# Clustered attention, mixture of experts and MLP: a new order of the work in the expert tiles

## The chip, the core and the metric

The kernel runs on one core of a Trainium2 chip. Its engines are TensorE (PE, matmuls and transposes), VectorE (DVE), ScalarE (ACT), GpSimd (POOL) and SyncE (SP), which here only issues DMAs. Each engine works through its own list of instructions in order, and semaphores tie the lists together. The metric is the time of one execution on the device in microseconds (us), as a median of several runs; lower is better.

## The reference

Three layers follow each other, all in float32.

```python
# 1. attention, B=2 H=8 S=768 D=64, 16 clusters: a query sees only keys of its own cluster
q_assign = argmax(einsum(q_n, c_n)); k_assign = argmax(einsum(k_n, c_n))
scores = where(q_assign[..., None] == k_assign[..., None, :], scale * q @ k.T, -1e9)
x = softmax(scores) @ v                  # -> (1536 tokens, 512)
# 2. mixture of experts, E=8, hidden 1024, one expert per token
e_idx = argmax(x @ w_gate, axis=1); gate_w = softmax(x @ w_gate)[e_idx]
eom = sigmoid(x @ w_output_gate)[e_idx]
for e in range(E):
    out[mask] = gate_w * eom * (maximum(x[mask] @ w1[e], 0) @ w2[e])
# 3. MLP, hidden 2048
h = out @ w_in
return (h * sigmoid(1.702 * h)) @ w_out
```

## The kernel before, in words

**Precision.** Each float32 operand of a large matmul is split into a high part in the fp32r format and a low part (the rest). One product is three matmuls: low times high, high times low, high times high. ScalarE (`*_high`, `high`, and `split_*` for weights) makes the high parts, VectorE (`*_low`, `low`, and its own `split_*`) the low ones.

**Attention** takes the first 296 us. It also computes the gate logits. As soon as the first batch's six columns of 128 tokens are done, they are given to experts; the other six follow in two stages of three columns at the end (`STAGES`). `choose(st, ...)` picks each token's expert on VectorE; `ranks(st)` on TensorE counts, with small bf16 matmuls (L785), how many tokens ahead of this one go to the same expert; `place(st)` on VectorE (L1441) turns that into the row `pos`. GpSimd then writes the rows of `x` to their places in DRAM, `xs` (`place_rows`, indirect DMAs), and token number and gate scale to `row_info` (`place_info`, L601). Every expert has a region of its own in `xs`.

**Tiles.** An expert's rows are worked on in tiles of 128. The numbers of tiles are known only at run time (`ntiles`). Since a region's last tile is not full, SyncE writes 128 rows of zeros behind its last row (`fill(e)`, L468); a fetch of rows by ScalarE for expert e + 1 waits for that expert's zeros (`s_pad`, L1169).

**The loop.** `expert_loop` (L345) writes out for each expert a body for its first tile (k = 0), one for its second (k = 1, under an If), and a loop for the further ones (k = 2, under an If). `only(e)` runs, in place of the second body, where an expert has one tile. TensorE, ScalarE, VectorE and SyncE each run this structure with their own `expert_tile(p, e, k)`. A call works at two tiles: it finishes tile p and starts tile g = p + 1.

On TensorE (L948) a tile is: `down(p, ., 0)` (6 matmuls of the second layer), `tile_transpose(g)` (4 transposes of the fetched rows `xg`), `down(p, ., 2)` (6), `hidden_transpose(p, 1)` (4 transposes of the hidden rows), a wait for `xtl_done`, `hidden(g, e, 0)` (12 matmuls), `down(p, ., 4)` and `(p, ., 6)` (12), `hidden_transpose(g, 0)` (4), `hidden(g, e, 1)` (12) and `turned(p)` (4 transposes of the scaled output).

On ScalarE (L1199) it is: two loads of row numbers, `tile_high(g)`, `fetch` of the rows after (a DMA), `high(p, 1)`, `relu(g, 0)`, two weight splits, `scaled(p)` (output times gate scale), `high(g, 0)`, two splits, `relu(g, 1)`, `turned_high(p)`. VectorE follows with the low parts (L1594). The splits are of the second weights of the same expert in the first tile, and of the first weights of the next expert in the second; `first_of_next` does the latter for an expert with one tile.

**Weights.** SyncE fetches 1 MB pieces into `raw`, which shares its memory with `wl`; in an expert's first tile it waits until the last tile of the expert before is through with its first weights (`h_ready`), then `fetch_first(e + 1)`, and until it is through with the second (`y_ready`), then `fetch_second(e + 1)` (L487). Before the loop SyncE does, in order: `fill(0)`, wait for the dispatch, rows of tile 1, `fill(1)`, wait for `g_rows` (the row numbers `tile_row`), `fetch_second(1)`, `fill(2)`.

**GpSimd** reads one tile's scales per tile from `row_info` (L675), the first after all of `place_info` has landed.

**The MLP** runs from about 532 us to the end in three groups of 512 tokens.

## Time and profile before

| | |
|---|---|
| median of 3 runs | 807.75 us (807.22 to 811.66) |
| the profiled execution | 811.05 us, its span 809.6 us |
| TensorE busy | 750.1 us, 93% of the span |
| VectorE, ScalarE, GpSimd busy | 425.4, 371.3, 164.5 us |
| chain that ended last | PE 70%, ACT 6%, DVE 6%, issue 4%, DMA 4%, SP queue 4%, POOL 3% |
| read from DRAM, written | 56.01 MB, 9.05 MB |

The profile lists every instruction with its engine and its line in the code. Matmuls overlap each other, so a matmul of 0.39 us that starts 0.23 us after the one before costs 0.23: read the distance between starts. Times in the rows are in us from the start of the span. A bracket after a row gives how long the engine had been idle and what it then waited for.

### The profile page before, as it was taken

Reading aid. Unit: us, or ns where it says so; the run is one execution under the profiler, and the core shown is the slowest. Engines: PE = TensorE matmul, PEld = TensorE weight load, DVE = VectorE, ACT = ScalarE, POOL = GpSimd, SP = SyncE. Lnnn points to the kernel's source line nnn. Section 1 sums busy time; section 2 is a strip of 40 time slices with the busy share of each in tenths; the row PEclk is TensorE's granted clock in tenths of the full one; section 3 lists DMA queues with packets and bytes.
Section 4 is the critical chain, followed back from the end, with each engine's and each line's share of the span. In section 5 each row is a group of like instructions: output and inputs, shape, how many; then the busy total and the mean of one; then the engine's idle time right before and its main releaser. Section 6 shows DMA issues by size and latency. Waiting matters only on the chain.

```text
span 809.6 us, 11950 instructions
## 1 busy us (share of the span) xinstructions
PE 750.1 (93%) x4099; PEld 640.2 (79%) x4099; DVE 425.4 (53%) x791; ACT 371.3 (46%) x707; POOL 164.5 (20%) x253
## 2 busy tenths in 40 slices
PE   4799999999999997679999999999999999999994
PEld 3699899988988875468777878878888888888883
DVE  4587888879878866246464646454322212221221
ACT  2577777777776854256565656463201110110110
POOL 5232242222625874101010101010000100020001
PEclk9999999999999999879999999999999999999998
DMA  8672552835526534864655465160000100010001
GB/s 178 149 173 67 133 124 64 185 70 132 138 68 138 211 116 120 248 236 140 238 179 188 136 217 209 39 208 2 1 0 7 46 0 1 1 53 0 1 1 52
DMA packets 61331, 86.36 MB, mean 107 GB/s; under 512 B 32577, under 2 KB 34769, under 8 KB 60753
## 3 DMA queue, kind: packets, MB, share of 16 engines
q1 hardware_dynamic: 55728, 75.23, 32.9%
q0 software_dynamic: 3376, 6.35, 2.2%
q10 hardware_dynamic: 2160, 3.93, 1.8%
q8 instruction: 38, 0.62, 0.3%
q14 instruction: 29, 0.23, 0.1%
HBM read 56.01 MB, written 9.05 MB: 80 GB/s over the span
## 4 chain that ended last, share of the span: by engine, by line
PE 70%; ACT 6%; DVE 6%; issue 4%; DMA 4%; SPq 4%; POOL 3%; ACTq 2%; another core or an unknown queue 0%; DVEq 0%; POOLq 0%
PE ps L982 16%; PE ps L697 8%; PE ps L997 5%; PE ps L998 5%; PE ps L999 5%; PE ps L770 4%; PE ps L912 4%; PE ps L914 3%; PE ps L913 3%; SPq L399 3%; PE ps L899 2%; PE ps L747 2%; PE ps L901 2%; PE ps L900 2%; PE ps L743 2%
## 5 line engine op out<-in xcount | busy, mean ns | idle before, releaser
L1375 DVE TENSOR_TENSOR pt_l<-ps,pt_h 128x384 fp32r<-128x384 f32 x192 | 105.9, 552 | 41.7 <-ACT pt_h L1086 40.5
L1244 ACT ACTIVATE g<-ps 128x512 f32<-128x512 f32 x48 | 28.7, 598 | 205.4 <-PE ps L982 205.4
L1628 DVE CAST gt_h<-g 128x512 fp32r<-128x512 f32 x48 | 20.5, 427 | 179.7 <-ACT g L1244 179.7
L1086 ACT CAST pt_h<-ps 128x384 fp32r<-128x384 f32 x192 | 92.6, 483 | 43.9 <-PE ps L697 43.8
L697 PE MATMUL ps<-ident,probs 128*128 128x128 f32 x576 | 97.3, 278 | 3.5 <-DVE pt_l L1375 1.9
L1334 DVE TENSOR_REDUCE nmax<-ps 128x1 f32<-128x768 f32 x96 | 91.0, 948 | 7.6 <-PE ps L747 7.6
L1057 ACT ACTIVATE probs<-ps,nmax 128x768 f32<-128x768 f32 x96 | 87.6, 913 | 4.8 <-DVE nmax L1334 4.8
L697 PEld LDWEIGHTS ps<-ident,probs 128*128 128x128 f32 x576 | 70.7, 144 | 17.6 <-DVE pt_l L1375 4.3
L982 PE MATMUL ps<-x2t_h,wl 128*128 128x512 f32 x192 | 74.9, 390 | 0.3 <-DVE wl L1545 0.3
L997 PE MATMUL ps<-wh,gt_l 128*128 128x512 f32 x192 | 74.8, 390 | 0.0
L982 PE MATMUL ps<-x2t_h,wh 128*128 128x512 f32 x192 | 74.7, 389 | 0.0
L999 PE MATMUL ps<-wh,gt_h 128*128 128x512 f32 x192 | 74.7, 389 | 0.0
L982 PE MATMUL ps<-x2t_l,wh 128*128 128x512 f32 x192 | 74.7, 389 | 0.0
L998 PE MATMUL ps<-wl,gt_h 128*128 128x512 f32 x192 | 74.7, 389 | 0.0
L770 PE MATMUL ps<-pt_h,vs 128*128 128x384 f32 x192 | 72.7, 379 | 0.0
L899 PE MATMUL ps<-wh,ht_l 128*128 128x512 f32 x128 | 54.9, 429 | 11.2 <-DVE ht_l L1497 6.1
L770 PE MATMUL ps<-pt_l,vs 128*128 128x384 f32 x192 | 64.7, 337 | 0.0
L912 PE MATMUL ps<-wh,xt_l 128*128 128x512 f32 x128 | 53.3, 416 | 7.0 <-DVE xt_l L1491 6.6
L743 PE MATMUL ps<-ka,qa 128*128 128x384 f32 x192 | 58.1, 384 | 1.2 <-DMA kb<-lo_t 1.2
L1545 DVE TENSOR_TENSOR wl<-raw,wh 128x1024 fp32r<-128x1024 f32 x36 | 42.6, 1221 | 25.6 <-ACT wh L1155 25.6
L1540 DVE TENSOR_TENSOR wl<-raw,wh 128x1024 fp32r<-128x1024 f32 x36 | 42.6, 1220 | 24.3 <-ACT wh L1150 24.1
L747 PE MATMUL ps<-kb,qb 80*128 80x384 f32 x192 | 50.8, 346 | 3.0 <-DMA kb<-onehot_t 3.0
(198 smaller groups left out, 1451.6 us busy)
## 6 DMA issues: line engine op xcount, KB each, us to landing
raw<-in_moe_w SPq DMA_DIRECT2D x32, 1024.0 KB, 7.9
ka<-hi_t SPq DMA_DIRECT2D x32, 192.0 KB
raw<-in_moe_w_in SPq DMA_DIRECT2D x4, 1024.0 KB, 5.8
raw<-in_moe_w_out SPq DMA_DIRECT2D x4, 1024.0 KB, 6.7
xg<-xs ACTq DMA_DIRECT2D x15, 256.0 KB
qn<-in_q SPq DMA_DIRECT2D x16, 192.0 KB, 3.6
kn<-in_k SPq DMA_DIRECT2D x16, 192.0 KB, 3.9
vn<-in_v SPq DMA_DIRECT2D x8, 384.0 KB, 5.0
```

What stands on the lines that cost most here:

```text
L697: return nc.tensor.transpose(dst, src, ident[0:src.shape[0], :] if src.shape[0] < P else ident[:, :])
L743: nc.tensor.matmul(ps[:, bank + half, 0:GQ], qa[par][h][:, rows], ka[par][h][:, half * GQ:(half + 1) * GQ], start=True, stop=False)
L770: last = nc.tensor.matmul(ps[:, 6, 0:GQ], vs[par][:, h * T + c, :], src[gp][:, c, :], start=(c == 0 and src is pt_h), stop=(c == T - 1 and ...
L912: nc.tensor.matmul(ps[:, half, :], xt_l[:, c, :], wh[slot][:, w], start=(c == 0), stop=False)
L982: last = nc.tensor.matmul(ps[:, f % 2, :], a[c // 2][:, w], b[:, c, cols], start=first, stop=(c == DC - 1 and a is wh and b is x2t_h))
L997: nc.tensor.matmul(ps[:, 4 + j, :], gt_l[f % 2][:, tok], wh[slot][:, w], start=(f == 0), stop=False)
L998: nc.tensor.matmul(ps[:, 4 + j, :], gt_h[f % 2][:, tok], wl[slot][:, w], start=False, stop=False)
L999: last = nc.tensor.matmul(ps[:, 4 + j, :], gt_h[f % 2][:, tok], wh[slot][:, w], start=False, stop=(f == FC2 - 1))
L1057: nc.scalar.activation(probs[s % 2][:, :].rearrange("p (a n) -> p a n", a=2), halves(score_bank(s)), ACT.Exp, bias=nmax[:, s % 4:s % 4 + 1 ...
L1086: nc.scalar.copy(pt_h[g % 2][:, half * GT:(half + 1) * GT, t3 * P:(t3 + 1) * P], ps[:, 4 + half, 0:GQ].rearrange("p (c n) -> p c n", c=GT) ...
L1334: nc.vector.reduce_max(nmax[:, s % 4:s % 4 + 1], halves(score_bank(s)), AX.XY, negate=True).then_inc(m_ready, 1)
L1375: nc.vector.tensor_tensor(pt_l[g % 2][at_p], ps[:, 4 + half, 0:GQ].rearrange("p (c n) -> p c n", c=GT), pt_h[g % 2][at_p].bitcast(F32), AL ...
```

## The change

- `expert_loop` has an argument `alike`. TensorE sets it: its k = 1 body goes, and one loop handles all tiles after an expert's first. The other engines keep their structure.
- In TensorE's tile `hidden_transpose(p, 1)` moves up behind `tile_transpose(g)`; `hidden_transpose(g, 0)` and `turned(p)` stand together in the middle of `hidden(g, e, 1)`. The two tiles ahead of the loop are reordered likewise. One more `tile_transpose` stands behind the loop.
- ScalarE and VectorE do `tile_high(g + 1)` and `tile_low(g + 1)` as the last operations of a tile, not the first; the weight splits and `turned_*` are placed anew.
- SyncE issues `fill(0)` to `fill(2)` together and every later one an expert earlier; `fetch_second(1)` no longer waits for `g_rows`.
- `ranks` counts only within a stage. What earlier stages add (and region start and gap) is carried in `offset` by VectorE and added in `place` as a second product.

```diff
-        def expert_loop(eng, counter, tile, only=None):
+        def expert_loop(eng, counter, tile, only=None, alike=False):
...
+                if e and not alike:
                     with eng.If(n > 1):
                         tile(eng.snap(counter), e, 1)
                         eng.reg_add(counter, counter, 1)
-                with eng.If(n > 2):
-                    with eng.Fori(2, n):
+                done = 1 if e and alike else 2
+                with eng.If(n > done):
+                    with eng.Fori(done, n):
                         tile(eng.snap(counter), e, 2)
                         eng.reg_add(counter, counter, 1)
...
             sp.wait_ge(g_filled, 1)
-            fill(0)
+            for e in range(3):
+                fill(e)
             sp.wait_ge(s_pad[0], 16)
             sp.wait_ge(s_disp, 16 * NT)
             sp.dma_start(xg[:, :], xs[TILE:2 * TILE, :]).then_inc(xg_in, 16)
-            fill(1)
             sp.wait_ge(pv_done, PAIRS * NG)
-            sp.wait_ge(g_rows, 1)
             fetch_second(1)
-            fill(2)
+            fill(3)
...
                 if k == 0:
-                    if e + 2 < E:
-                        fill(e + 2)
+                    if e + 3 < E:
+                        fill(e + 3)
...
-                nc.tensor.matmul(dst, ones[:, :], region_b[:, 0:n, :].rearrange("p t e -> p (t e)"), start=True, stop=False)
-                if st:
-                    nc.tensor.matmul(dst, ones[0:1, :], gap_b[0:1, :, :].rearrange("p t e -> p (t e)"), start=False, stop=False)
-                for d in range(a + n - 1, 0, -1):
-                    skip = max(0, d - a)
-                    nc.tensor.matmul(dst[:, skip * E:], ones[:, :], picked[:, (a + skip - d) * E:(z - d) * E], start=False, stop=False)
-                nc.tensor.matmul(dst, before[:, :], picked[:, a * E:z * E], start=False, stop=True).then_inc(g_rank, 1)
-                if st != 1:
-                    for t in range(z):
...
+                nc.tensor.matmul(dst, before[:, :], picked[:, a * E:z * E], start=True, stop=False)
+                for d in range(1, n):
+                    last = nc.tensor.matmul(dst[:, d * E:], ones[:, :], picked[:, a * E:(z - d) * E], start=False, stop=(d == n - 1))
+                last.then_inc(g_rank, 1)
+                for t in range(a, z):
+                    last = nc.tensor.matmul(total_of(st), ones[:, :], pick_b[:, t, :], start=(t == a), stop=(t == z - 1))
+                last.then_inc(g_total, 1)
...
             hidden(0, 0, 0, 3)
-            hidden(0, 0, 1, 0, 1)
+            hidden(0, 0, 1, 0, 2)
             hidden_transpose(0, 0)
-            hidden(0, 0, 1, 1)
+            hidden(0, 0, 1, 2)
             down(0, 0, 0)
             hidden_transpose(0, 1)
             down(0, 0, 2)
             down(0, 0, 4)
+            tile_transpose(1)
             down(0, 0, 6)
-            turned(0)
-            tile_transpose(1)
             pe.wait_ge(xtl_done, 2)
             hidden(1, 0, 0)
-            hidden(1, 0, 1, 0, 1)
+            hidden(1, 0, 1, 0, 2)
             hidden_transpose(1, 0)
-            hidden(1, 0, 1, 1)
+            turned(0)
+            hidden(1, 0, 1, 2)
...
                 g, ep = p + 1, e if k else e - 1
                 down(p, ep, 0)
                 tile_transpose(g)
+                hidden_transpose(p, 1)
                 down(p, ep, 2)
-                hidden_transpose(p, 1)
                 pe.wait_ge(xtl_done, g + 1)
                 hidden(g, e, 0)
                 down(p, ep, 4)
                 down(p, ep, 6)
+                hidden(g, e, 1, 0, 2)
                 hidden_transpose(g, 0)
-                hidden(g, e, 1)
                 turned(p)
-
-            expert_loop(pe, tiles, expert_tile)
+                hidden(g, e, 1, 2)
+
+            expert_loop(pe, tiles, expert_tile, alike=True)
...
             down(last, E - 1, 0)
+            tile_transpose(total)
             down(last, E - 1, 2)
...
                 row, ahead_row = row_at(p + 1), region_row_of(g + 1)
-                tile_high(g)
                 fetch(ahead_row, min(e + 1, E - 1))
                 high(p, 1)
-                relu(g, 0)
                 if k < 2:
                     split(whose, 0)
                     split(whose, 1)
+                relu(g, 0)
+                if k < 2:
+                    split(whose, 2)
                 scaled(p)
                 high(g, 0)
+                turned_high(p, row)
                 if k < 2:
-                    split(whose, 2)
                     split(whose, 3)
                 relu(g, 1)
-                turned_high(p, row)
+                tile_high(g + 1)
...
                 row = row_at(p + 1)
-                tile_low(g)
                 low(p, 1)
                 if k < 2:
                     split(whose, 0)
                     split(whose, 1)
+                    split(whose, 2)
                 low(g, 0)
+                turned_low(p, row)
                 if k < 2:
-                    split(whose, 2)
                     split(whose, 3)
-                turned_low(p, row)
+                tile_low(g + 1)
```

Ahead of the loop ScalarE and VectorE are reordered in the same sense: `tile_high(1)` stands before `scaled(0)`, `tile_low(1)` before the gates, and `tile_high(2)`, `tile_low(2)` at the end.

## Rows read from the trace of the kernel before

**Rows 1.** The page, part 1: busy us, share of the span, instructions.

```profile
PE 750.1 (93%) x4099; PEld 640.2 (79%) x4099; DVE 425.4 (53%) x791; ACT 371.3 (46%) x707; POOL 164.5 (20%) x253
```

**Rows 2.** Timeline of TensorE, 320 to 376: start, us, engine, line, operation, output, input, shape, count.

```profile
339.95 0.80 PE L899 MATMUL ps<-wh,ht_l 128*128 128x512 f32 x1 [6.06 <-DVE ht_l L1497]
...
345.24 0.82 PE L697 MATMUL ps<-ident,h 128*128 128x128 f32 x4
...
354.24 0.77 PE L899 MATMUL ps<-wh,ht_l 128*128 128x512 f32 x1 [4.98 <-issue]
...
369.00 0.60 PE L697 MATMUL ps<-ident,y 128*128 128x128 f32 x4
```

**Rows 3.** Timeline of ScalarE, 270 to 385.

```profile
338.59 0.58 ACT L1145 CAST ht_h<-ps 128x512 fp32r<-128x512 f32 x1 [8.47 <-DMA xs<-zeros]
```

**Rows 4.** Timeline of SyncE's DMA issues, 270 to 560.

```profile
310.68 0.35 SPq L477 DMA_DIRECT2D xg<-xs  x1
...
320.65 0.93 SPq L440 DMA_DIRECT2D raw<-in_moe_w  x2
322.48 4.23 SPq L471 DMA_DIRECT2D xs<-zeros  x2
```

**Rows 5.** DMA queues in 350 to 352: queue, packets, MB, share.

```profile
q8 instruction: 1, 0.02, 3.0%
```

**Rows 6.** Timeline of VectorE: start of the experts, expert 1's end, a steady tile.

```profile
311.95 0.69 DVE L1497 TENSOR_TENSOR ht_l<-ps,ht_h 128x512 fp32r<-128x512 f32 x1 [2.15 <-ACT ht_h L1145]
...
314.47 1.22 DVE L1540 TENSOR_TENSOR wl<-raw,wh 128x1024 fp32r<-128x1024 f32 x1
...
350.94 4.63 DVE L1540 TENSOR_TENSOR wl<-raw,wh 128x1024 fp32r<-128x1024 f32 x4
...
413.28 0.69 DVE L1491 TENSOR_TENSOR xt_l<-ps,xt_h 128x512 fp32r<-128x512 f32 x1 [2.05 <-ACT xt_h L1134]
```

**Rows 7.** Windows of 5 us: length, busy time of each engine, granted clock, DMA share, GB/s.

```profile
340.00:345.00 5.00, 5.00 (x12) 3.98 (x13) 2.36 (x2) 1.55 (x2) 0.74 (x2) 0.50 0.60 239
```

**Rows 8.** Timeline of TensorE, steady tiles and the last ones.

```profile
378.73 0.39 PE L901 MATMUL ps<-wh,ht_h 128*128 128x512 f32 x1
378.96 0.60 PE L697 MATMUL ps<-ident,h 128*128 128x128 f32 x4
379.31 0.48 PE L912 MATMUL ps<-wh,xt_l 128*128 128x512 f32 x1
379.63 0.40 PE L913 MATMUL ps<-wl,xt_h 128*128 128x512 f32 x1
...
399.54 0.60 PE L697 MATMUL ps<-ident,h 128*128 128x128 f32 x4
...
410.86 0.60 PE L697 MATMUL ps<-ident,xg 128*128 128x128 f32 x4
...
414.03 0.50 PE L912 MATMUL ps<-wh,xt_l 128*128 128x512 f32 x1 [0.75 <-DVE xt_l L1491]
...
529.02 0.60 PE L697 MATMUL ps<-ident,y 128*128 128x128 f32 x4
...
534.52 0.50 PE L982 MATMUL ps<-x2t_h,wl 128*128 128x512 f32 x1 [0.32 <-DVE wl L1545]
```

**Rows 9.** Timeline of ScalarE, 378 to 427.

```profile
400.18 0.59 ACT L1145 CAST ht_h<-ps 128x512 fp32r<-128x512 f32 x1 [0.71 <-PE ps L697]
...
409.75 0.59 ACT L1160 CAST x2t_h<-ps 128x512 f32 x1
412.66 0.58 ACT L1134 CAST xt_h<-ps 128x512 fp32r<-128x512 f32 x1 [2.32 <-issue]
```

**Rows 10.** Timeline of TensorE, 293.5 to 320.

```profile
319.21 0.50 PE L912 MATMUL ps<-wh,xt_l 128*128 128x512 f32 x1 [1.62 <-DVE xt_l L1491]
```

**Rows 11.** Timeline of GpSimd, 270 to 385.

```profile
339.60 0.59 POOL L675 DMA_DIRECT2D scale<-row_info  x1 [14.54 <-issue]
```

**Rows 12.** DMA issues of the whole span: count, KB each, median us to landing.

```profile
scale<-row_info POOLq DMA_DIRECT2D x16, 1.0 KB, 4.1
```

More of the change, by code:

```diff
@@ L97, in clustered_attention_moe_mlp @@
         first_rows = sb("first_rows", [P, 2, NROWS])
-        region_b = sb("region_b", [P, T, E], BF16)
+        offset = sb("offset", [P, 3, E])
         thresholds = sb("thresholds", [P, NTHR])
@@ L269, in clustered_attention_moe_mlp @@
         g_count = sem("g_count")
+        g_offset = sem("g_offset")
         g_first = sem("g_first")
@@ L1182, in _ @@
             high(0, 1)
-            for i in range(1, 4):
-                split_first(1, i)
+            split_first(1, 1)
+            tile_high(1)
             scaled(0)
+            act.wait_ge(g_region, 1)
+            fetch(region_row_of(2), 1)
+            split_first(1, 2)
+            relu(1, 0)
+            high(1, 0)
             act.wait_ge(s_disp, 16 * NT)
             turned_high(0, 0)
-            tile_high(1)
-            act.wait_ge(g_region, 1)
-            fetch(region_row_of(2), 1)
-            relu(1, 0)
-            high(1, 0)
+            split_first(1, 3)
             relu(1, 1)
+            tile_high(2)
             act.wait_ge(g_tiles, 1)
@@ L1237, in _ @@
             wait_apart(act, xg_in, 16 * total + 16)
-            wait_apart(act, xtl_done, total)
+            wait_apart(act, xtl_done, total + 1)
             for m in range(NMG):
@@ L1436, in total @@
             def total(st):
-                dve.wait_ge(g_total, 1 + st // 2)
-                nc.vector.tensor_copy(count[:, 1:SEG], ps[:, 7, TOTAL:TOTAL + E]).then_inc(g_count, 1)
+                dve.wait_ge(g_total, st + 1)
+                if st < 2:
+                    nc.vector.tensor_tensor(offset[:, st + 1, :], offset[:, st, :], total_of(st), ALU.add).then_inc(g_offset, 1)
+                if st:
+                    nc.vector.tensor_tensor(count[:, 1:SEG], count[:, 1:SEG], total_of(st), ALU.add).then_inc(g_count, 1)
+                else:
+                    nc.vector.tensor_copy(count[:, 1:SEG], total_of(st)).then_inc(g_count, 1)
             def place(st):
@@ L1445, in place @@
                 bank, at_c = (5, (st - 1) * GT * E) if st else (7, 3 * P)
+                if st:
+                    dve.wait_ge(g_offset, st)
+                    dve.wait_ge(g_first, 1)
+                dve.wait_ge(g_pick, st + 1)
+                nc.vector.tensor_tensor(rank[:, own, 1, :], offset[:, st, :].unsqueeze(1).to_broadcast([P, n, E]), pick_b[:, own, :], ALU.mult)
                 dve.wait_ge(g_rank, st + 1)
@@ L1462, in first_gap @@
                 link(nc.vector.tensor_scalar(gap[:, 1:2], gap[:, 0:1], 0.0, None, ALU.max), g_step)
-                nc.vector.tensor_copy(gap_b[:, :, 0:1], gap[:, 1:2].unsqueeze(1).to_broadcast([P, GT, 1])).then_inc(g_first, 1)
+                nc.vector.tensor_tensor(offset[:, 1, 0:1], offset[:, 1, 0:1], gap[:, 1:2], ALU.add).then_inc(g_first, 1)
             def gate(b, part):
@@ L1574, in _ @@
             split_first(1, 0)
+            tile_low(1)
+            split_first(1, 1)
             gate(1, 0)
             gate(1, 1)
-            turned_low(0, 0)
-            tile_low(1)
             dense_rows()
-            split_first(1, 1)
             split_first(1, 2)
             low(1, 0)
+            turned_low(0, 0)
             split_first(1, 3)
+            tile_low(2)
             dve.wait_ge(g_tiles, 1)
```

20 lines of the change are left out of this document (9 added, 11 removed).

## The prediction

> **What bounds the kernel now.** I read the page first. TensorE is busy for 93% of the span [rows 1], so the time is TensorE's own work plus the places where it waits, and only those two can change. The windows and the timeline of TensorE over the experts (296 to 534 us) then show three kinds of lost time.
>
> First, two holes early on: 6.06 us before the matmul at 339.95 and 4.98 us before the one at 354.24 [rows 2]. The first is a chain through a DMA. TensorE wants ht_l from VectorE, which wants ht_h from ScalarE, and ScalarE stood 8.47 us at the fetch of the next rows, held by the zero rows that pad expert 2's region [rows 3]. SyncE issued that pad at 322.48, behind the 2 MB of expert 1's second weights, which went out at 320.65 because they waited for tile_row [rows 4]. The second hole is put down to "issue": VectorE and ScalarE had delivered (down(2,1,0) needs ht_l of tile 2 and the first half piece of w2), yet nothing started. Inside it, in 350 to 352 us, one packet went through the instruction queue [rows 5]. At this point expert 1 ends with one tile: VectorE's four w1 splits in a row at 350.94 [rows 6] are first_of_next, which only a one-tile expert runs. TensorE then jumps over two written-out tile bodies, k = 1 and k = 2. After every other expert it jumps over one, and I see no hole there.
>
> Second, what the holes do to the clock: in 340 to 345 the granted clock is 0.50 [rows 7], the 1.2 GHz level, and had been 1.00 before TensorE stood idle. The twelve matmuls from 339.95 to the transposes at 345.24 [rows 2] took 0.44 us each in place of 0.23; after the second hole it is the same for about 4 us.
>
> Third, each steady tile waits for xt_l: 0.75 us in the tile of 410.86 [rows 8]. ScalarE began that tile's xt_h 1.80 us after the transposes began, with 2.32 us of "issue" before it [rows 9]: it first loads two row numbers and takes the branches. Where it is ready (ht_h at 400.18 for transposes at 399.54) it starts after 0.64 us.
>
> **Part 1, pads and w2 ahead.** fill(1), fill(2) go before the wait for the dispatch, and fetch_second(1) follows xg of tile 1 (310.68) at about 311.5 in place of 320.65, no longer waiting for tile_row [rows 4]. All fills that the first fetches need are then 15 us old, so the 6.06 us and the half clock behind it go. Added: two pads of 256 KB among the six indirect writes of rows; at the traffic's pace they delay the end of the dispatch by 0 to 1 us. They cost nothing, since tile 1 is limited by VectorE (part 3); without that cover it would be up to 1.
>
> **Part 2, one further-tile loop on TensorE.** Expert 1 now skips one body, as the others do without a hole, so the 4.98 us and its half clock go. Expert 7 has three tiles (16 in all: 2, 1, five times 2, 3) and now jumps back once. No row shows a jump back over a body. The loop's exit at 529.02 has no gap [rows 8], so 0 is one end, and the 4.98 us the other; the DMA engines are idle at that moment, which is nearer the first: I take 1.5.
>
> The Trainium skill, "Runtime: NRT & Kernel Launch", section on instruction fetch mechanics, says that prefetch is sequential and that a taken branch whose target is not in the two-page window waits for a DMA of the page. The trace agrees at 354.24. Read against the change, the same rule would charge a jump back too, and every loop entry whose target has not been brought in: rival C.
>
> **Part 3, start of the experts.** tile_transpose(1) moves ahead of down(0,0,6), tile_high(1) ahead of scaled(0), tile_low(1) ahead of the gates. Before, hidden(1,0) started at 319.21 after 1.62 us of waiting for xt_l [rows 10]. VectorE becomes its limit: low(0,1) at 311.95, the region rows until the split at 314.47, which takes 1.13 [rows 6], then tile_low, whose start comes 0.75 before the matmul (413.28 to 414.03). That is 314.47 + 1.13 + 0.75 = 316.35. About 0.5 comes off because ranks(2) has 6 small matmuls in place of 26 and hT(0,0) sits three matmuls later, behind relu: 315.8, a gain of 3.4. The bounds are 1.6 (only the wait) and 4.5. Ranks: 37 small matmuls of stages 1 and 2 become 12. The new VectorE operations (offset, count, the second product) are some six of under 0.2 us; about 0.5 in all, charged below.
>
> **Part 4, from hidden(1,0) to the end of hidden(3).** Before: 369.00 − 319.21 = 49.8 us [rows 2, 10]. After, on TensorE alone: 120 matmuls of 0.23 (378.73 to 378.96) = 27.6. A group of four transposes takes 0.35 (378.96 to 379.31), and the first matmul behind it 0.32 in place of 0.23, 0.09 more [rows 8]. Joined, eight cost 0.70 + 0.09 = 0.79; five such pairs make 3.95. Sum 31.5. What is late next is the one-tile expert: its four w1 splits for expert 2 now stand behind tile_high(3), which waits for transposes in the next tile. From these transposes at T: xt_h starts at T + 0.64, VectorE's first split ends near T + 3.4, the others 1.16 apart (4.63 for four, [rows 6]), and ht_l of half 1 comes at T + 8.0, behind the splits and the row numbers on ScalarE. TensorE would want it at T + 4.9 and waits 3.2 in small pieces (2.5 to 5). So 34.7 us, a gain of 15.1.
>
> **Part 5, steady tiles.** Before: (529.02 − 369.00)/12 = 13.34 us [rows 2, 8]. Without waits it would be 48 × 0.23 + 4 × 0.44 = 12.8. After: 11.04 + 2 × 0.79 = 12.62 plus waits. The joining itself gives only 0.18. The waits come from the order: tile_high and tile_low are now the last things of a tile, before the row numbers and branches. The chain from the transposes is 0.64 + 0.62 + 0.75 = 2.01 (the last two: 412.66 to 413.28 to 414.03); TensorE has 0.70 + 0.09 + 6 × 0.23 = 2.17 to do meanwhile: no wait, by 0.16. Behind ScalarE's row numbers now stands high(p,1): start of the loads T + 0.64, 2.9 us from one to the next as between 409.75 and 412.66 [rows 9], the fetch, then ht_h and ht_l end at about T + 5.0 against T + 4.9 wanted: 0.1 a tile. 13.34 − 12.72 = 0.6, times 12 = 7.4 (bounds 2.2, the joins alone, and 8.6).
>
> **Part 6, the tail.** tile_transpose(total) is extra and takes the place that turned had at the tile's end: even on TensorE. But ScalarE now does tile_high(total) before the four w2 splits of the last expert weights, 1.3 us later than before, and TensorE already waits 0.32 for these at 534.52 [rows 8]. I take 1.3 (0 to 2).
>
> **Part 7, scales.** scaled(1) needs row_info, written by six indirect DMAs. The last was out at 325.06 and the next POOL instruction came 14.54 us later, at 339.60 [rows 11]; a scale then takes 4.1 to land [rows 12]. That was covered by the holes that now go. After: the gates end about 1.2 later, the sixth write goes out at 326.2, but expert 1's w2 is through by then and only expert 2's w1 (from 322) stands beside it. Scale lands at 331 to 337; turned(1) wants y at 332.7. A wait of 0 to 5, taken as 1.5.
>
> The Trainium skill, "DMA: Bandwidth & Descriptors", section on queues, rings and completion order, has a DMA engine take turns between queues packet by packet, so small writes should not wait for megabytes on another queue. The 14.54 us speak against relying on that; by the rule part 7 would be 0 and the forecast 1.5 lower.
>
> **Sum**, against the profiled execution's own 811.05 (span 809.6 and 1.45 around it): −3.4 − 15.1 − 7.4 + 1.5 (jump back) + 1.3 + 1.5 + 0.5 = −21.1, so 790. The median of before is 807.75, 3.3 below the profiled one. Runs differ by how long the DMA-bound holes last, I think, and after has none of these, so I keep 790: 17.8 under the median.
>
> **Rivals.** (A) Late scales: row_info again lands only when weight traffic ends, near 337 to 339. turned(1) waits 6 us and the clock halves for 2.5 more: about 7 above part 7's 1.5, 797. For it: the 14.54. Against: half the traffic is gone.
> (B) Tiles keep their wait: the margin is 0.16, and ScalarE is not ready after three splits and relu. Then only the joins count, 5.2 less gain: 795.
> (C) The other side, slower than before: TensorE's loop makes every entry or exit of the body wait for instructions. Place: the start and end of the loop at seven experts, where the page's rule of part 2 would put it. The price is up to the 4.98 us of 354.24 with its 2.5 of half clock, 7.5; it turns the sign from 21 / 7 = 3 us per expert on. At 4 us: 790 + 28 = 818. For it: loops in place of straight code. Against: the loop at 515.85 to 529.02, entered and left, shows no gap.
> (D) The change doesn't reach its aim: the second hole was traffic, not the jump, and stays: 7.5 more, 797.
>
> **Chances.** Forecast 0.58, A 0.15, B 0.12, C 0.04, D 0.11. The range 781 to 801 holds about 0.85; its low end is all bounds good (part 5 at 8.6, no jump-back, tail or scale cost, a shorter one-tile wait). No change is within 0.5%, 4 us, what a measurement of this kernel can tell: 0.02. Slower 0.04, faster 0.94.
>
> **What would show it.** No wait of ScalarE for the zero rows; no TensorE idle above 2 us at the end of expert 1; hidden(1,0) near 316; TensorE at 1.00 clock through 320 to 360; steady tiles at 12.7 with the wait for xt_l under 0.1; an issue gap of 1 to 2 us between the second and third tile of expert 7. Wrong would be a new wait of turned(1) for y, or tiles at 13.1 and more.

## The result, and the profile after

The kernel after takes 803.62 us (median of 11 runs, 800.72 to 806.54), the kernel before 809.01 (11 runs, 807.22 to 811.66): a ratio of 0.9931, 95% interval 0.9914 to 0.9948. The direction is the predicted one, but the gain is less than a third of what was forecast: 5.4 us between the medians, against 17.8. 790 was forecast, and 803.62 lies above the range's 801. The profiled execution of after took 800.72 us (span 799.2), 10.3 less than the profiled one of before. Those 10.3 flatter the change: 800.72 is the fastest of after's eleven, and 811.05 is 2 us above the median of before. What follows explains the profiled pair; the slower executions of after have no trace.

The page after, part 1 (busy us, share of the span, instructions), against [rows 1]:

```profile
PE 744.7 (93%) x4077; PEld 638.1 (80%) x4077; DVE 428.6 (54%) x798; ACT 371.1 (46%) x708; POOL 165.9 (21%) x252
```

The timeline of TensorE after, 310 to 525, against [rows 2, 8, 10]:

```profile
343.96 1.11 PE L700 MATMUL ps<-ident,y 128*128 128x128 f32 x4 [10.29 <-ACT y L1176]
...
352.28 0.47 PE L911 MATMUL ps<-wh,xt_l 128*128 128x512 f32 x1 [1.15 <-DVE wl L1554]
...
357.09 0.50 PE L898 MATMUL ps<-wh,ht_l 128*128 128x512 f32 x1 [0.54 <-DVE ht_l L1511]
...
361.35 0.60 PE L700 MATMUL ps<-ident,h 128*128 128x128 f32 x4
361.79 0.60 PE L700 MATMUL ps<-ident,y 128*128 128x128 f32 x4
362.14 0.48 PE L911 MATMUL ps<-wh,xt_l 128*128 128x512 f32 x1
362.46 0.40 PE L912 MATMUL ps<-wl,xt_h 128*128 128x512 f32 x1
...
363.60 0.39 PE L898 MATMUL ps<-wh,ht_l 128*128 128x512 f32 x1
...
383.00 0.50 PE L898 MATMUL ps<-wh,ht_l 128*128 128x512 f32 x1 [0.24 <-DVE ht_l L1511]
...
524.23 0.51 PE L983 MATMUL ps<-x2t_h,wl 128*128 128x512 f32 x1 [1.37 <-DVE wl L1559]
```

The two holes of before are gone, and a single longer one stands in their place: turned(1), the transposes of tile 1's scaled output y, waits 10.29 us for y. ScalarE and GpSimd in the same stretch name the chain behind it, which is that of [rows 11, 12]:

```profile
343.22 0.69 ACT L1176 ACTIVATE y<-ps,scale 128x512 f32<-128x512 f32 x1 [11.81 <-DMA scale<-row_info]
```

```profile
318.27 0.96 POOL L604 DMA_INDIRECT row_info<-token_info,pos  x1 [10.23 <-DVE token_info L1493]
...
325.81 0.96 POOL L604 DMA_INDIRECT row_info<-token_info,pos  x1 [0.30 <-issue]
338.14 0.59 POOL L678 DMA_DIRECT2D scale<-row_info  x1 [11.37 <-issue]
```

token_info (token number and gate scale) is ready at 318.0; six writes of row_info are issued in 8.5 us, one after another; the read of the scales goes out 11.4 us after the last; y comes 5 us after that. Before, the read went out at 339.60 [rows 11]. So this chain is only 1.5 us ahead of where it was, and most of what TensorE gained ahead of it turned into waiting. The granted clock then falls to the 1.2 GHz level, as in [rows 7]; over 10 us its mean is 0.60 (windows; columns as there):

```profile
335.00:345.00 10.00, 1.04 (x5) 1.04 (x6) 0.59 (x1) 1.16 (x2) 1.14 (x2) 0.60 0.71 241
```

What the DMA engines did meanwhile, after, in 322 to 324, in 324 to 326, in 326 to 328 and in 328 to 330 (queue: packets, MB, share of 16 engines; a packet counts where it starts; q1 carries SyncE's transfers, q0 GpSimd's):

```profile
q1 hardware_dynamic: 16, 0.07, 174.3%
q0 software_dynamic: 21, 0.00, 0.9%
```

```profile
DMA packets 0, 0.00 MB, mean 0 GB/s; under 512 B 0, under 2 KB 0, under 8 KB 0
```

```profile
q1 hardware_dynamic: 128, 0.52, 77.3%
```

```profile
q1 hardware_dynamic: 216, 0.82, 100.6%
q0 software_dynamic: 81, 0.00, 3.0%
```

Sixteen packets of the weight queue, as many as there are engines, took 2 × 16 × 1.743 / 16 = 3.49 us each. While they were under way no other packet started on any queue for the 2 us from 324 to 326, although SyncE had begun to issue w1 of expert 2 at 321.93. From 326 on a packet of the same 4 KB took 2 × 16 × 0.773 / 128 = 0.19 us. A row write makes 32 packets on q0. The first two writes had started theirs before 324 (43 packets in 320 to 322 and 21 in 322 to 324); the other four, 128 packets, started only from 328 on, the last of them after 333. The slow packets came right behind the first two row writes.

The whole path in one table, in us between TensorE's own marks: the first transposes of xg, the first matmul of hidden(1,0), the transposes of xg for tiles 4 and 15, the last transposes of y, the end. Between the marks TensorE has the same work in all kernels but for one group of four transposes, 0.44 us, in two places: turned(0) counts to the front in before, e1 and e2 and to the early part in the others, and the extra tile_transpose is in the tail of the others. The parts and the span are those of the one profiled execution, the median is over all; each ratio is against the executions of before that were timed with that kernel, whose medians lay between 807.97 and 810.16.

```
kernel               to xg  front  early  11 tiles  tail   rest   span   median, ratio [95%]
before              295.41  23.80  51.62  146.84   23.78  268.15  809.6  809.01
after               295.31  19.94  49.71  141.41   24.79  268.04  799.2  803.62  0.9931 [0.9914, 0.9948]
e1 pads only        296.01  24.55  43.08  146.46   23.78  268.12  802.0  803.81  0.9935 [0.9913, 0.9957]
e2 loop only        296.61  24.63  50.41  146.62   23.79  268.14  810.2  809.69  0.9998 [0.9979, 1.0018]
e3 gates early      295.96  29.08  37.60  141.38   24.79  268.09  796.9  799.07  0.9889 [0.9866, 0.9911]
e4 weights held     296.77  20.07  47.68  141.39   24.78  268.11  798.8  800.17  0.9897 [0.9872, 0.9921]
e5 wide rows        296.03  20.31  45.39  141.51   24.81  268.15  796.2  797.38  0.9853 [0.9832, 0.9875]
e6 spaced           296.34  20.00  61.16  141.41   24.84  268.15  811.9  814.23  1.0064 [1.0042, 1.0086]
e7 wide, early      295.35  29.22  37.70  141.47   24.82  268.14  796.7  799.41  0.9881 [0.9863, 0.9900]
e8 no loop          294.47  19.99  50.19  141.43   24.87  268.15  799.1  802.36  0.9916 [0.9899, 0.9934]
e9 wide, gates mid  295.85  20.83  37.78  141.98   24.91  268.15  789.5  790.84  0.9771 [0.9752, 0.9790]
e10 wide, held      297.15  20.25  42.91  141.97   24.87  268.15  795.3  794.04  0.9815 [0.9797, 0.9833]
e11 wide, gates rows 295.41 20.75  37.67  141.43   24.81  268.13  788.2  790.88  0.9781 [0.9763, 0.9799]
e12 gates rows      295.65  20.54  39.93  141.41   24.84  268.13  790.5  794.74  0.9834 [0.9802, 0.9866]
e13 e11, no loop    295.98  20.80  37.80  141.96   24.92  268.14  789.6  790.06  0.9776 [0.9763, 0.9790]
e14 e11, apart      296.25  20.83  37.75  141.83   24.85  268.09  789.6  790.44  0.9783 [0.9769, 0.9796]
e15 writes later    294.70  20.18  37.68  141.48   24.84  268.12  787.0  788.92  0.9767 [0.9752, 0.9782]
```

### The profile page after: what moved, and what is told of

It reads as the page before. It is cut to its first block, busy times and chain, and to the rows that moved or that the text cites. A ratio compares the mean times of both kernels' runs of the same rounds, so it can differ in the third digit from the quotient of the medians.

```text
span 799.2 us, 11904 instructions
## 1 busy us (share of the span) xinstructions
PE 744.7 (93%) x4077; PEld 638.1 (80%) x4077; DVE 428.6 (54%) x798; ACT 371.1 (46%) x708; POOL 165.9 (21%) x252
## 4 chain that ended last, share of the span: by engine, by line
PE 78%; issue 5%; DVE 4%; ACT 4%; DMA 3%; POOL 2%; SPq 2%; ACTq 1%; POOLq 0%; DVEq 0%
PE ps L983 16%; PE ps L700 11%; PE ps L773 6%; PE ps L998 5%; PE ps L999 5%; PE ps L1000 5%; PE ps L898 3%; PE ps L750 3%; PE ps L899 3%; PE ps L900 3%; PE ps L746 3%; PE ps L912 3%; PE ps L911 3%; PE ps L913 3%; PE ps L726 2%
## 5 line engine op out<-in xcount | busy, mean ns | idle before, releaser
L1511 DVE TENSOR_TENSOR ht_l<-ps,ht_h 128x512 fp32r<-128x512 f32 x32 | 22.1, 691 | 74.7 <-ACT ht_h L1146 73.9
L898 PE MATMUL ps<-wh,ht_l 128*128 128x512 f32 x128 | 52.4, 410 | 1.9 <-DVE ht_l L1511 1.9
L689 POOL DMA_INDIRECT out<-zeros,row_token x3 | 3.0, 994 | 245.6 <-ACT zeros L1258 157.6
```

## The experiments

**e1, the pads alone** (before, with SyncE's order of after):

```diff
-            fill(0)
+            for e in range(3):
+                fill(e)
...
-            fill(1)
-            sp.wait_ge(g_rows, 1)
             fetch_second(1)
-            fill(2)
+            fill(3)
```

> The kernel before with SyncE's part of the change alone: fills 0 to 2 together, later fills one expert earlier, the second weights of expert 1 right after the rows of tile 1. Theory S (what gave the gain back is the scale of tile 1, which lands late whatever TensorE does): the 8.47 us wait of ScalarE for the zero rows goes, but scaled(1) then waits for its scale until about 343 to 345, so y of tile 1 comes as late as before (345.56) and the 4.98 us hole behind it stays: ratio to before 0.997 to 1.002. Theory of the forecast (pads are the whole cause of the first hole, the scale costs 1.5 us): the 6.06 us hole and its 2.4 us of half clock go, less 1.5, about 802, ratio 0.991.

The timelines of TensorE, ScalarE and GpSimd in e1:

```profile
347.96 0.76 PE L898 MATMUL ps<-wh,ht_l 128*128 128x512 f32 x1 [5.48 <-issue]
```

```profile
339.38 0.69 ACT L1174 ACTIVATE y<-ps,scale 128x512 f32<-128x512 f32 x1 [0.72 <-DMA scale<-row_info]
```

```profile
334.69 0.59 POOL L674 DMA_DIRECT2D scale<-row_info  x1 [8.36 <-issue]
```

ScalarE's wait for the zero rows and TensorE's first hole are gone, the second stays: the pads did what was predicted. The ratio lies between those of the two theories (0.991, and 0.997 to 1.002). Theory S had y as late as before; it came at 339.38. So SyncE's new order alone brought the read of the scales forward by 4.9 us, to 334.69, 8.36 us after the last write in place of 14.54. In the whole change most of that is lost again. There TensorE is through with its weights sooner, SyncE starts w1 of expert 2 at 321.93, beside the row writes, and the read goes out at 338.14; in e1 w1 starts at 328.51, behind them. One part of the change alone gives as much as the whole change (0.9935 against 0.9931).

**e2, the loop alone** (before, with `alike=True` for TensorE).

> The kernel before with TensorE's single further-tile loop alone. Theory J (the 4.98 us at 354.24 is the jump over two bodies, which needs instructions that are not at hand): the hole goes, and the next limit is the one-tile expert's splits, hidden(3) near 356.4 in place of 360.25: 4 us less, with no gap at the jump back in expert 7: ratio 0.995. Theory T (the hole is traffic of the weights on the DMA engines, whatever the jump): the hole stays, ratio 1.000. If loops cost instructions at each expert: slower than before.

The timeline of TensorE in e2:

```profile
341.95 0.80 PE L901 MATMUL ps<-wh,ht_l 128*128 128x512 f32 x1 [5.96 <-DVE ht_l L1499]
...
358.65 0.79 PE L914 MATMUL ps<-wh,xt_l 128*128 128x512 f32 x1 [4.17 <-DVE xt_l L1493]
```

The "issue" hole of 4.98 us is gone, and 4.17 us of waiting for xt_l stand in its place. So the hole did come from the jump over two bodies, but under it VectorE was late too. There is no gain (0.9998; 0.995 was expected).

**e3, gates early** (after, with `gate(1, 0)` and `gate(1, 1)` right behind `filled`, 13 us earlier).

> The kernel after with gate(1, 0) and gate(1, 1) moved on VectorE from behind split_first(1, 1) to right behind filled, into 2.4 us in which VectorE is idle. The six writes of row_info then go out from about 308 in place of 318. Theory S: they land by about 320, the scale by 326, turned(1) does not wait: the 10.29 us and 1.8 us of half clock go, 12 us below after, about 791.5, ratio to before 0.979. Theory I (GpSimd's 11.4 us of 'issue' before the scale is its own instruction fetch at the loop, not the landing): the scale still goes out at 338, ratio 0.993 as after. If the writes themselves slow down whatever else is in flight: the slow stretch moves to 310 to 320, where the second weights of expert 1 and the rows of tile 2 are fetched; these have some 7 us to spare, so 791 to 796.

The wait for y is gone and the early part falls to 37.6. By part 4's own marks (hidden(1,0) to the end of hidden(3)) that is 36.2, where part 4 without a wait has 34.7. But the front grows by 9 us. ScalarE in e3:

```profile
311.29 0.60 ACT L1142 ACTIVATE h<-ps 128x512 f32<-128x512 f32 x1 [4.20 <-remote]
318.44 0.58 ACT L1146 CAST ht_h<-ps 128x512 fp32r<-128x512 f32 x1 [6.56 <-remote]
```

TensorE's transposes for that ht_h had started at 311.94, 6.5 us before. GpSimd has 14.15 us before its read here too, but that is no longer the landing of the writes: it also waits for tile_row, which VectorE, held up behind ScalarE, writes at 327.24, and the read goes out 3 us later.

**e4, weights held** (after, SyncE fetches w1 of expert 2 only when all row writes have landed: `sp.wait_ge(s_info, 16 * NT)` before `fetch_first(e + 1)`).

> The kernel after, where SyncE waits for the landing of all row_info writes before each fetch of first weights (that holds only the one for expert 2). Theory W (the writes land late because 2 MB of weights stand in the queues beside them): last write out at 326.8, landed by 329, scale by 333, turned(1) waits under 1 us: about 10 us below after, ratio 0.981; expert 2's first weights arrive near 337, before they are wanted at about 345. Theory S2 (the writes are slow by themselves, or held by something else than those weights): the scale lands at 337 or later, turned(1) waits as before, and the weights come later too: ratio 0.993 or worse.

The read went out at 336.67 and the wait was 7.22 us instead of 10.29, with the last write issued at 327.40. The idle time of GpSimd before the read is 8.31 us, as in e1, where no weights stood beside the writes either, and 11.37 in after. The weight traffic makes 3 us of it; the rest stands without any.

**e6, spaced** (after, each of the last six row writes waits for the one before, by `pool.wait_ge(s_info, 16 * t + 16)` behind each).


> The kernel after, where each of the six last row_info writes waits until the one before has landed. It measures one write's landing by itself: the distance of two issues. Theory B (each write occupies the engines for microseconds): distances of 4 us and more, the scale out after 345, slower than after by 5 us or more, ratio to before 1.00 or above. Theory D (only a crowd of writes is slow): distances of 2.5 to 3 us, no packet above 1 us on the other queues, scale out near 338 to 340 as after: ratio 0.993 to 0.996.

The timeline of GpSimd in e6:

```profile
323.90 1.42 POOL L604 DMA_INDIRECT row_info<-token_info,pos  x1 [3.59 <-DMA row_info<-token_info,pos]
331.15 1.04 POOL L604 DMA_INDIRECT row_info<-token_info,pos  x1 [5.83 <-DMA row_info<-token_info,pos]
336.66 0.96 POOL L604 DMA_INDIRECT row_info<-token_info,pos  x1 [4.47 <-DMA row_info<-token_info,pos]
344.00 0.96 POOL L604 DMA_INDIRECT row_info<-token_info,pos  x1 [6.38 <-DMA row_info<-token_info,pos]
```

The DMA issues of e6, 319 to 353 (count, median us to landing):

```profile
row_info<-token_info,pos POOLq DMA_INDIRECT x6, 4.8
```

A write of 128 rows of 8 bytes, 1 KB in all, leaves GpSimd waiting 3.2 to 6.4 us for its landing; the last, with nothing beside it, landed 2.8 us after its issue, and the read went out 2.9 us after that. So some 3 us of every idle time before the read are GpSimd's own. TensorE waits 21.84 us for y, and the time is above that of before: a microsecond in this chain is about a microsecond of the kernel (11.55 us more of waiting, 12.7 more of span).

**e5, wide rows** (after, with rows of 64 bytes in row_info, so 8 KB a write; the reads take the first 8 bytes of each, and the zeros that fill row_info at the start come in four DMAs in place of one).

```diff
-    row_info = nc.dram_tensor("row_info", (E * REGION + TILE, 2), F32, kind="Internal").ap()
+    row_info = nc.dram_tensor("row_info", (E * REGION + TILE, 16), F32, kind="Internal").ap()
```

> The kernel after with rows of row_info 64 bytes long in place of 8 (token_info has 16 columns, 14 of them zero; the zeros at the start come in four DMAs). In five traces so far the first packets beside or behind the six writes of row_info took 2.6 to 4 us in place of 0.1, wherever the writes stood. Theory B (writes of 8 bytes, eight rows to a 64-byte line, hold the DMA engines): with whole lines the long packets go, the sixth write lands by 329 in place of about 335, the scale goes out by 332 in place of 338, y near 336 in place of 343.2: TensorE's 10.29 us hole shrinks to 3 and the clock stays at 1.00; 794 to 796, ratio to before 0.983. Theory C (any scatter of 768 rows does it, or the weights beside it): as after, 0.993.

GpSimd, TensorE, and the DMA queues in 323 to 325, in e5:

```profile
333.83 0.59 POOL L683 DMA_DIRECT2D scale<-row_info  x1 [5.98 <-issue]
```

```profile
340.50 1.12 PE L705 MATMUL ps<-ident,y 128*128 128x128 f32 x4 [5.77 <-ACT y L1181]
```

```profile
q1 hardware_dynamic: 27, 0.11, 46.6%
```

Eight times the bytes, and the read goes out 5.4 us sooner after the last write. The first weight packets behind the writes take 2 × 16 × 0.466 / 27 = 0.55 us each instead of 3.49. The number of writes and the traffic beside them are those of after, so the short rows make this stall. Other short transfers still do it in e5: behind the next tile's scales, 128 times 8 bytes, the weight packets that start in 345 to 346 take 16 × 1.278 / 8 = 2.56 us.

```profile
q1 hardware_dynamic: 8, 0.03, 127.8%
```

Only these two widths were run. Why the short rows hold the engines, and at what width that ends, no run shows.

**e7, wide rows and gates early** (e5 and e3 together).

> Both: rows of 64 bytes and the gates moved ahead (as in the run with the early gates). Theory B: the front keeps its 19.9 us (28.5 to 29 with the early gates and short rows), and the part from hidden(1,0) to tile_transpose(4) its 37.6: 295.3 + 19.9 + 37.6 + 141.4 + 24.8 + 268.0 = 787 of span, 788.5 us, ratio to before 0.974. Theory C: the front still loses 9 us, 799, ratio 0.988.

The early part is 37.7 again and the front 29.2 again. Theory B failed: the front's 9 us are not made by the rows' size.

**e8, no loop** (after, TensorE without `alike=True`).

> The kernel after with TensorE's loop undone (bodies for k = 1 and k = 2 again, as before). If the jump over two bodies costs what the trace of before shows (4.98 us of 'issue') and nothing hides it: a hole behind expert 1's tile, up to 5 us and half clock more than after, 806 to 809, ratio to before 0.997 to 1.000. If the one-tile expert's weight splits hide it, as the null result of the loop alone says for the kernel before: 803 to 804, ratio 0.993, with an 'issue' hole and a shorter wait for wl or xt_l in its place.

Nothing changes (0.9916 against 0.9931), and no "issue" hole comes back. TensorE stands 9.78 us for y shortly before the jump; that this covers what the jump costs is a guess, no row shows it.

**e9 and e11, wide rows and the gates in the middle**: behind low(0,1) in e9, behind region_rows in e11.

```diff
             region_rows()
+            gate(1, 0)
+            gate(1, 1)
             split_first(1, 0)
             tile_low(1)
             split_first(1, 1)
-            gate(1, 0)
-            gate(1, 1)
```

> Kernel after, with 64-byte rows in row_info, and with both parts of gate(1) put on VectorE behind low(0,1) and ahead of region_rows. Theory S (the scales' chain is what the early part waits for): token_info is ready at about 312.1 instead of 318, the six row writes are issued 312.5 to 320.7, the scales' read goes out at about 328 (333.8 with 64-byte rows alone), y of tile 1 is there before turned(1) wants it at 334, so TensorE's 5.8 us wait and the 1.7 us of half clock behind it go: early part 38 us, front 20 to 21, span about 789. Rival J (row writes issued ahead of about 318 hold ScalarE up, as with the gates right behind filled, where it stood 4.2 and 6.6 us with no releaser on the chip): early part 38, but front 24 to 29, span 793 to 797. If the span stays at 796 with y in time, something else sets the early part.

> Kernel after with 64-byte rows in row_info, and both parts of gate(1) on VectorE behind region_rows, ahead of the first split of expert 1 (about 4 us earlier than there, 2 us later than in the kernel with them behind low(0,1)). Theory S: token_info at about 314, scales' read out at about 330, y at 335.5, TensorE's wait 1 to 2 us, early part 39.5 to 41, front 20 to 21.5 (the split of expert 1 and the eviction of tile 1 come up to 1.6 us later on VectorE), span about 791. Rival J: front longer by some us in proportion to how early the row writes start, 22 to 25, span 794 to 796.

GpSimd, ScalarE and TensorE in e11:

```profile
314.65 1.69 POOL L609 DMA_INDIRECT row_info<-token_info,pos  x1 [6.24 <-DVE token_info L1498]
...
327.54 0.59 POOL L683 DMA_DIRECT2D scale<-row_info  x1 [4.40 <-issue]
```

```profile
332.93 0.69 ACT L1181 ACTIVATE y<-ps,scale 128x512 f32<-128x512 f32 x1 [0.59 <-PE ps L905]
```

```profile
329.79 0.50 PE L903 MATMUL ps<-wh,ht_l 128*128 128x512 f32 x1 [0.63 <-DVE ht_l L1516]
...
341.20 0.47 PE L916 MATMUL ps<-wh,xt_l 128*128 128x512 f32 x1 [1.17 <-DVE wl L1559]
...
346.01 0.50 PE L903 MATMUL ps<-wh,ht_l 128*128 128x512 f32 x1 [0.53 <-DVE ht_l L1516]
```

ScalarE now finds the scales there and waits for TensorE's sum instead. With y in time the early part is 37.7 and the front 20.8, and the kernel takes 790.9, with the change otherwise as it is. Theory S held in both; the read was out some 2 us sooner than it expected.

**e10, wide rows and weights held** until the scales of tile 1 have landed.

> Kernel after with 64-byte rows in row_info, and SyncE fetching w1 of expert 2 only once the scales of tile 1 have landed. Theory W (the 2 MB of w1[2] beside the scales' read make its 5.5 us and some of the row writes' landing): scales' read out at about 332.5 and landed 2 to 3 us later, y of tile 1 at about 336.5 against 339.8, TensorE's wait 2.5 us instead of 5.8, early part 42, span about 793, less 1 if w1[2] then comes late for its split. Rival (the read takes its 5 us with nothing beside it, as a DMA of 128 rows of 8 bytes): y at 338 to 339, early part 44 to 45, span 795 to 796.

y came at 334.86, sooner than expected, and TensorE's wait for it is gone. But it then waits for what was held. TensorE in e10:

```profile
344.98 0.47 PE L917 MATMUL ps<-wh,xt_l 128*128 128x512 f32 x1 [3.69 <-DVE wl L1560]
...
348.71 0.79 PE L917 MATMUL ps<-wh,xt_l 128*128 128x512 f32 x1 [1.35 <-DVE wl L1560]
```

So the weights cost this chain some 6 us in e5: from the read to y it took 5.9 us there and 1.9 here, and from the last write to the read 5.98 and 4.08. But they can't be held: net 3 us worse than moving the gates. Beside e4 this is the plainest comparison of the two row sizes. In both no weights stand beside the writes, and the read goes out 8.31 us after the last write with 8-byte rows, 4.08 with 64-byte rows.

**e12, the gates' place alone** (after with e11's move of the gates, 8-byte rows).

> Kernel after as it is, 8-byte rows in row_info and all, with both parts of gate(1) on VectorE behind region_rows: the place of the gates alone, without the wide rows. Theory S: the chain starts 3.8 us earlier (token_info at 314.2 instead of 318.0), the scales' read goes out at about 334, y of tile 1 comes at about 339.4, TensorE's wait for it is 6 to 7 us instead of 10.3, early part 44.5 to 46, span about 795. Rival N (the 8-byte rows' stall of the DMA engines starts with the writes, so an earlier start also holds up the rows of tile 1 and ScalarE): front 22 to 25 instead of 19.9, span 797 to 799. Rival P (the stall comes only where w1[2] and the row writes meet, and an earlier start gets most writes done before it): read out at 328 to 330 as with wide rows, no wait for y, span 789 to 791.

The profiled execution had the read out at 330.18 and 0.38 us of waiting for y, as rival P said (span 790.5). But that was the fastest of its five times, which lie between 791.93 and 799.34, where e11's lie between 789.67 and 792.48. That the stall of the short rows comes back in the slower ones is likely, and not shown: they have no trace. By the ratios the two parts together give 12 us. The place of the gates gives 8 of them if it comes first (e12) and 6 if it comes after the wide rows (e5, e11).

**e13 and e14, two parts undone in e11**: TensorE without the loop (e13); turned(p) three matmuls behind hidden_transpose(g, 0), so that these two groups stand apart (e14).

> The fastest kernel so far (64-byte rows, gates behind region_rows), with TensorE's expert loop as in before: k = 1 written out, and two bodies jumped over at the end of expert 1. Theory L (the jump over two bodies makes TensorE wait for instructions, the 4.98 us of before with its half clock): an idle time of about 5 us put down to issue near 340 to 347, early part 43 to 45, span 794 to 796. Rival T (the hole of before was not the jump, or the jump is covered by the weight splits that TensorE waits for there anyway): early part 37.7 to 38.5, span 788 to 789.

> The fastest kernel so far (64-byte rows, gates behind region_rows), with turned(p) three matmuls later than hidden_transpose(g, 0) in TensorE's tile, so that the two groups of four transposes no longer stand together. Theory N (a group costs 0.44 us beside its matmuls, joined or not, as the trace of after shows with 0.44 from one group's start to the next): 12.85 to 12.87 us a tile as before, same time within 0.3 us. Rival P (as predicted, joining spares 0.09 a pair): 12.95 a tile, 1.1 to 1.3 us longer over the tiles. Third: turned later makes turned_high and turned_low, and the splits behind them, 0.7 us later, which TensorE could see as waits for ht_l or wl: over 0.1 a tile and named in its brackets.

TensorE in e13:

```profile
341.74 0.50 PE L903 MATMUL ps<-wh,ht_l 128*128 128x512 f32 x1 [1.69 <-issue]
```

The jump over two bodies shows again, as 1.69 us, and stands in place of the 1.17 us for wl. On the whole it costs nothing (37.80 against 37.67). In e14 a tile takes 12.89 us; e11 has 12.86 and e9, with the same tiles as e11, 12.91. So standing together spares a pair of groups nothing that these runs can tell, at most 0.04 us.

**e15, gates early, writes later** (e7, with GpSimd holding the row writes until region_rows is done: `pool.wait_ge(g_region, 1)`).

> The kernel with 64-byte rows and the gates right behind filled (front 29.2, early 37.7, span 796.7), where GpSimd additionally holds the six row writes until VectorE has done region_rows, at about 312.5. The gates' own work stays early. Theory J (the row writes issued right behind the six indirect writes of rows hold ScalarE up): front back to 20 to 21, scales' read out at about 326, no wait for y, early 37.7, span about 788. Rival G (the gates on VectorE, 1.7 us ahead of low(0,0), and what they set off cause the long front): front stays at 28 to 29 and the span at 796.

The front is back at 20.18, with the gates as early as in e7 and only the writes moved from 308.7 to 312.3. So the row writes in flight between 309 and 316 held ScalarE up there, not the gates. This kernel has the lowest median, 788.92 us, 0.9767 of before, and 1.6% less than after by the two ratios; its interval overlaps those of e9, e11, e13 and e14. Shorter stops of ScalarE with the same releaser stand in most of the traces, at the end of the six indirect writes of rows of x: 1.75 us in after, 2.30 here. How a write holds up ScalarE, which in that stretch waits for TensorE alone, no row shows: the releaser is given as "remote". That stays open.

## Why the prediction was wrong, step by step

**Part 7, scales: the step that failed.** "A wait of 0 to 5, taken as 1.5" was 10.29 us of idle and 1.7 of matmuls at the lower clock, 12.0. The sixth write went out as said (325.81 against 326.2) and y was wanted as said (at 333.5 against 332.7). What was mis-sized is the time from that write to the scale: "lands at 331 to 337" had the read out by 333 at the latest, and it went out at 338.14. Rival A had the mechanism and too low a price, 6 us of wait.

Its sentence against ("half the traffic is gone") is right about the traffic and wrong in what it makes of it. With only that half gone, in e1, the 14.54 us of [rows 11] were 8.36, so traffic was a good part of them. But a read 8.4 us after the last write is still too late for TensorE at 333.5. And in the whole change w1 of expert 2 meets the short rows: 3 us more (e4), with the stall of all engines behind them. With 64-byte rows the 11.37 us are 5.98 (e5). That the small writes are slow by themselves was no term of the sum.

With hidden(1,0) at 315.25 and hidden(3) ending at 363.60, part 4's stretch took 48.35 us against 34.7 + 1.5 predicted, 12.1 over. 10.5 of that is this wait; the other 1.6 is in part 4 and part 5's price of the joins, below. With the chain moved out of the way, e11 and e15 came to 790.9 and 788.9 against the forecast's 790. That shows what was missing. That they come so close is partly luck: the errors of the other terms nearly cancel.

The Trainium skill, "DMA: Bandwidth & Descriptors", was used in the prediction for engines taking turns between queues. Its section on back-pressure in remote DMA says, of transfers between cores, that stalled writes also stall the source engine's other queues. The trace of after looks like that in kind, although these writes go to DRAM: sixteen packets of 3.49 us on the weight queue, and no other packet started beside them from 324 to 326. That the cause is the same, no run shows.

**Part 1, pads.** Right: no wait for zero rows, and e1 gives 8.5 us of early part for it.

**Part 2, loop.** The jump back was taken as 1.5; there is no gap in expert 7, cost 0. The 4.98 us credited to the loop were worth nothing by themselves: e2 has a wait for xt_l underneath, e13 a wait for wl. The hole was what the prediction said it was, the jump; the step left out what was late next below it. Rival D, that the hole was traffic, is excluded by e2. Rival C did not come: TensorE shows no gap at any expert's loop. The trace shows 4.98 and 1.69 us for the jump over two bodies, and no gap for the jump back. By the Trainium skill, "Runtime: NRT & Kernel Launch", section on instruction fetch mechanics, only a branch whose target lies outside the two-page window waits. The missing gap agrees with that if the loop's start was still in the window, which no run shows.

**Part 3, start.** Predicted 315.8, measured 315.25. Right; e3 shows how little it takes to lose it.

**Part 4, what is late next.** The one-tile expert was predicted as 3.2 us of small waits. It is right: from the transposes at 348.70 to the wait at 357.09 the brackets are 1.15, 0.17, 0.17 and 0.54, and ht_l comes 8.4 us after the transposes, T + 8.0 predicted and 4.9 without waits. One wait of 0.62 for ht_l in tile 1, at 328.86, was not foreseen; with the slower start behind it, it costs 0.8. The joins cost 0.09 more a pair than taken, 0.45 for five. That is most of the 1.6.

**Part 5, steady tiles.** Predicted 12.72, measured 141.41 / 11 = 12.86 against 13.35: 5.9 us over twelve tiles, not 7.4. The waits for xt_l are gone, as said, so rival B did not come. The term of the joins was wrong: a pair takes 361.35 to 361.79, 0.44, then 0.35 and 0.09 more for the matmul behind it, 0.88, which is twice what one group took in [rows 8], and e14 confirms it. The wait for ht_l, taken as 0.1 in every tile, is 0.24 and 0.28 in two of them (at 383.00 and 408.91) and below that in the others.

**Part 6, tail.** Predicted 1.3, measured 1.05: the wait for wl grew from 0.32 to 1.37.

**The sum.** −3.96 start, −1.4 early with the scales in it, −5.95 tiles, +1.06 tail, −0.1 the rest: −10.35, and 811.05 − 800.72 = 10.33. The forecast of −21.1 missed by 12.2 in the early part and 1.45 in the tiles, and was too careful by 2.9 in the others (start, jump back, tail, small operations). This is the sum of the profiled pair; the medians are only 5.4 us apart, and where the other 5 us go no trace shows.

**Executions.** The argument that after would have no DMA-bound hole, so that its runs would not differ, failed with the step: they lie 5.8 us apart, those of e15 2.1.

## What to carry to other kernels

When a change shortens the path to a point, list every other chain that ends at that point and subtract its present end from the new time of need. Here the scale of tile 1 landed at about 339.6 + 4.1 = 343.7 before [rows 11, 12], and y would be wanted at 332.7. As long as nothing in the change is shown to make the scale earlier, 11 us of waiting can be read off before any run. An unexplained wait (14.54 us for 1 KB writes) is to be taken over as it stands until something shows how much of it goes with its supposed cause: traffic was part of it and not all.

A faster engine also moves the transfers that it triggers. Here it brought w1 of expert 2 forward by 6.6 us (321.93 against 328.51 in e1), onto the row writes that TensorE would then wait for. And a hole is worth only what is not late underneath it.

## What the runs showed of the hardware that was not expected

- Scattered writes of 8-byte rows to DRAM, 128 rows at a time: each landed 2.8 to 7.1 us after its issue, median 4.8 (e6). Weight packets behind them took 3.49 us instead of 0.19 (after). With rows of 64 bytes, eight times the data, these packets took 0.55 us, and the read went out 5.4 us sooner after the last write (e5). With no weights beside the writes it went out 8.31 and 4.08 us after (e4, e10).
- The same kernel varies by 7.4 us with 8-byte rows (e12) and by 2.8 with 64-byte rows (e11), five executions each. But e3, with 8-byte rows, varies by 2.6 (six executions), so the width alone does not make the spread.
- Row writes queued right behind six larger indirect writes go with two stops of ScalarE, of 4.20 and 6.56 us in e3. With their start 3.7 us later (e15 against e7) the front is 9 us shorter.
- A jump over two written-out tile bodies cost TensorE 4.98, 5.48 and 1.69 us in three kernels (before, e1, e13) and showed no gap in e8; the jump back of a loop over one body cost none.
- Two groups of four transposes cost 0.88 us together and 0.44 each apart.
